# An attention and two mixtures of experts on one core: the first mixture in tiles of 400 rows with the weights stationary

## What is computed

```python
# attention: B=2, H=8, S=768, D=64; queries see only keys of their hash bucket
x = attn_out.transpose(0, 2, 1, 3).reshape(1536, 512)

# first mixture: 8 experts, w1 [8,512,1024], w2 [8,1024,512], the best two for each row
noisy = x @ w_gate + log1p(exp(x @ w_noise)) * noise
top2, top2_w = two best of noisy, their softmax
for e in range(8):
    h = maximum(x[rows of e] @ w1[e], 0)
    out[rows of e] += top2_w * (h @ w2[e])

# second mixture: the same sizes, the best one for each row, fed with the first one's output
```

## Time and profile before

| | |
|---|---|
| median of 3 runs | 950.83 us (947.76 to 951.78) |
| profiled execution | 954.72 us |
| its span, first to last instruction | 953.0 us |
| PE busy | 862.1 us (90%), 4678 matmuls |
| PEld busy | 735.0 us (77%) |
| DVE, ACT, POOL busy | 580.4, 372.7, 399.2 us |
| DMA | 175.12 MB, mean 184 GB/s |

### The profile page before, as it was taken

The page is one execution under the profiler, slowest core; times in us unless marked ns, Lnnn a source line. Parts: engine busy times, 40 slices in busy tenths (PEclk is TensorE's granted clock), DMA queues, the critical chain, the costliest instruction groups (busy, mean ns, idle before and its releaser), DMA issues.

```text
span 953.0 us, 17167 instructions
## 1 busy us (share of the span) xinstructions
PE 862.1 (90%) x4678; PEld 735.0 (77%) x4679; DVE 580.4 (61%) x996; ACT 372.7 (39%) x625; POOL 399.2 (42%) x292
## 2 busy tenths in 40 slices
PE   3899999999984779999999999999886999999991
PEld 2788888888884558888888888887685888888870
DVE  4999999999986834444444444442637544444440
ACT  2778787777883013211112120210431344333003
POOL 2010110101222788642525161644316989896104
PEclk9999999999998779999999999999977899999996
DMA  6678669667884677442525251525586768784118
GB/s 150 134 228 244 163 173 272 207 136 224 250 318 164 212 265 233 166 164 80 173 87 177 67 193 70 175 87 150 149 288 210 274 211 262 224 262 155 44 33 276
DMA packets 101977, 175.12 MB, mean 184 GB/s; under 512 B 35712, under 2 KB 37760, under 8 KB 101952
## 3 DMA queue, kind: packets, MB, share of 16 engines
q1 hardware_dynamic: 66880, 82.79, 29.4%
q10 hardware_dynamic: 28672, 71.05, 23.0%
q0 software_dynamic: 6400, 20.98, 6.6%
HBM read 98.18 MB, written 57.15 MB: 163 GB/s over the span
## 4 chain that ended last, share of the span: by engine, by line
PE 80%; DVE 8%; issue 3%; another core or an unknown queue 3%; DMA 2%; ACT 2%; DVEq 0%; POOLq 0%; POOL 0%; ACTq 0%; SPq 0%
PE bank L1427 8%; PE bank L1429 8%; PE bank L1447 8%; PE bank L1428 8%; PE bank L1449 8%; PE bank L1448 8%; PE bank L1252 7%; PE bank L1458 3%; PE bank L1240 3%; PE bank L1263 3%; PE bank L1264 3%; PE bank L1241 3%; PE bank L1279 2%; PE bank L1409 2%
## 5 line engine op out<-in xcount | busy, mean ns | idle before, releaser
L549 POOL TENSOR_TENSOR wring<-stage,wring 128x1024 f32 (+1 forms) x116 | 274.3, 2401 | 177.7 <-ACT wring L748 171.4
L748 ACT ACTIVATE wring<-stage 128x1024 f32 (+1 forms) x116 | 121.1, 1059 | 372.5 <-PE bank L1429 119.0
L1427 PE MATMUL bank<-wring,xT_hl 128*128 (+1 forms) x352 | 145.3, 413 | 8.3 <-DVE xT_hl L1127 5.8
L1447 PE MATMUL bank<-wring,hT_hl 128*128 (+1 forms) x352 | 142.1, 404 | 4.1 <-DVE hT_hl L1145 4.1
L1429 PE MATMUL bank<-wring,xT_hl 128*128 (+1 forms) x352 | 140.8, 400 | 1.5 <-issue 1.5
L1428 PE MATMUL bank<-wring,xT_hl 128*128 (+1 forms) x352 | 140.8, 400 | 0.0
L1152 DVE COPY work<-bank 128x512 f32<-128x512 f32 x44 | 30.5, 692 | 180.8 <-PE bank L1449 164.5
L1449 PE MATMUL bank<-wring,hT_hl 128*128 (+1 forms) x352 | 138.3, 393 | 0.9 <-issue 0.9
L1448 PE MATMUL bank<-wring,hT_hl 128*128 (+1 forms) x352 | 137.8, 391 | 0.5 <-issue 0.5
L1134 DVE TENSOR_SCALAR work<-bank 128x512 f32<-128x512 f32 x88 | 60.7, 691 | 107.7 <-PE bank L1429 95.7
L890 DVE TENSOR_TENSOR wring<-bank,wring 128x768 fp32r<-128x768 f32 x96 | 91.9, 957 | 11.1 <-ACT wring L666 9.2
(11 more groups left out here) (181 smaller groups left out, 1389.5 us busy)
## 6 DMA issues: line engine op xcount, KB each, us to landing
stage<-in_moe_w_dram ACTq DMA_DIRECT2D x128, 512.0 KB
wring<-wring SPq DMA_DIRECT2D x92, 192.0 KB
ys<-work SPq DMA_DIRECT2D x44, 256.0 KB
work<-xs SPq DMA_DIRECT2D x38, 256.0 KB
xs<-stage SPq DMA_DIRECT2D x8, 1024.0 KB, 5.1
ys<-stage SPq DMA_DIRECT2D x7, 1024.0 KB, 7.2
xs<-stage SPq DMA_DIRECT2D x7, 512.0 KB, 7.9
ys<-stage SPq DMA_DIRECT2D x7, 512.0 KB, 8.0
```

The source lines that it names most:

```text
L549: nc.gpsimd.tensor_tensor(wring[:, bass.ds(at + DC * F, GW)], stage[:, at_stage(g, j), :], wring[:, bass.ds(at, GW)].bitcast(F32), ALU.sub ...
L748: nc.scalar.activation(wring[:, bass.ds(parity * SLOT + high_at(j), GW)], stage[:, j % STAGES, :], ACT.Copy).then_inc(w_high, 1)
L1427: mm(o, xT_hl[:, 0, c, :], wh, start=c == 0, stop=False)
L1447: mm(y_ps[:], hT_hl[:, 0, c, :], wh, start=c == 0, stop=False)
```

## The change

The first mixture gets loops of its own (`wide_experts` on PE and DVE, `wide_load` and `wide_store` on SP). The second keeps its tiles of 128.

- A tile is up to 400 rows of one expert, in blocks of 128, 128, 128 and 16. Rows stand in `xs` and `ys` without gaps; a tile's start row is read from the table `row_of`. What a tile computes beyond its expert's rows is overwritten by the next tile.
- The weights are stationary and the rows move, 400 columns a matmul, in both layers. `up` gives h already turned, so `turn_h` goes. `down` gives y turned, so four transposes for each block (`turn_y`) bring it back, in between the parts of the next `up`.
- In the last tile `down_rows` works block by block with h stationary, 512 columns a matmul, so that the blocks are stored one after the other.
- The ring is three halves (one layer of one expert each); the fourth half's place holds h and x.
- TensorE's code is written out for each of the 8 experts, each with a second copy of the step under a condition, for an expert of more than 400 rows.
- `tables(0)` moves behind the whole first `up`. PE, SP and ACT wait for it there. `gate_weights(0)` moves ahead of it. The first fetches stand at scatters 1, 5, 5 and 5.
- SP loads a whole tile's x with two DMAs, after the four stores of the tile before in its queue; each store waits for the landing of the one before.

In the diff, `wide_load` and `wide_store` are SP's, `high_part` is ACT's, `h_split` and the first `step` DVE's, `up` and the second `step` PE's. `y_out` copies 400 columns of turned y out of PSUM, `x_split` makes high and low of a block, `y_rows` copies 512 columns of y out of PSUM, `down(t, d)` makes 24 matmuls of 400 columns. `XS_TILES` and `YS_TILES` are 28 tiles for the first mixture, before 32 and 31.

```diff
+    WIDE = 400
+    BLOCKS = [min(P, WIDE - at) for at in range(0, WIDE, P)]
+    XS_TILES = [-(-(TOPK[0] * TOK + WIDE) // P), NT[1] + 1]
+        BACK_AT = (1, 3, 5, 6)
-                fetch_at = ((1, 5, 7, 9), (1, 4, 5, 6))[m]
+                fetch_at = ((1, 5, 5, 5), (1, 4, 5, 6))[m]
...
+            def wide_load(t):
+                row = wide_start(t)
+                sp.wait_ge(wide_xmm, t * NB)
+                sp.dma_start(work[:, 3 * DM:6 * DM].rearrange("p (b n) -> p b n", n=DM),
+                             xs_d[0][bass.ds(row, 3 * P)].rearrange("(b p) n -> p b n", p=P)).then_inc(wide_ld, 16)
+                sp.dma_start(wide_rows[3][0:BLOCKS[3]],
+                             xs_d[0][bass.ds(row + 3 * P, BLOCKS[3])]).then_inc(wide_ld, 16)
+            def wide_store(t):
+                row = wide_start(t)
+                for b, n in enumerate(BLOCKS):
+                    sp.wait_ge(wide_yrow, t * NB + (b + 2))
+                    if not (isinstance(t, int) and t == 0 and b == 0):
+                        sp.wait_ge(y_st, t * (16 * NB) + 16 * b)
+                    sp.dma_start(ys_d[0][bass.ds(row + b * P, n)], wide_y[b % 2][0:n]).then_inc(y_st, 16)
+            sp.wait_ge(xs_put, 16 * TT * TOPK[0])
+            sp.wait_ge(rt_tab, 1)
+            wide_load(1)
+            wide_store(0)
+            with sp.Fori(2, NTMIN[0]) as t:
+                wide_load(t)
+                wide_store(t - 1)
...
-            with act.Fori(2, E - 1) as g:
-                high_part(0, g, g, g % 2, table(0, g - 2))
+            for e in range(2, E):
+                high_part(0, e, (downed(e - 2), upped(e - 1)))
...
+                def h_split(t, f):
+                    dve.wait_ge(wide_upped, t * FC + (f + 1))
+                    src = wide_up[f % 3][:, 0:WIDE]
+                    vec.tensor_scalar(wide_h[0][:, f], src, 0.0, None, ALU.max).then_inc(wide_hhigh, 1)
+                    dve.wait_ge(wide_hhigh, t * FC + (f + 1))
+                    vec.scalar_tensor_tensor(out=wide_h[1][:, f], in0=src, scalar=0.0, in1=wide_h[0][:, f].bitcast(F32),
+                                             op0=ALU.max, op1=ALU.subtract).then_inc(wide_hrdy, 1)
+                def step(t, before):
+                    for d in range(DC):
+                        if d == DC - 1:
+                            x_split(t, d)
+                            y_out(before, d)
+                        else:
+                            y_out(before, d)
+                            x_split(t, d)
+                    for f in range(FC):
+                        h_split(t, f)
+                        if f in BACK_AT:
+                            b = BACK_AT.index(f)
+                            y_rows(before, b, wide_back, wide_backed, before * NB + (b + 1))
...
+                def up(t, f, at):
+                    to = wide_up[f % 3][:, 0:WIDE]
+                    for c in range(DC):
+                        high, low = weights(at + (c * F + f * P), P)
+                        mm(to, high, wide_x[0][:, c], start=c == 0, stop=False)
+                        mm(to, high, wide_x[1][:, c], start=False, stop=False)
+                        ins = mm(to, low, wide_x[0][:, c], start=False, stop=c == DC - 1)
+                def step(t, e, before, e_before):
+                    pe.wait_ge(w_low, e_before * GRAN + GRAN)
+                    for d in range(DC):
+                        down(before, d, at)
+                        if d < DC - 1:
+                            turn_x(t, d)
+                        if d == DC - 2:
+                            turn_x(t, d + 1)
+                    pe.wait_ge(w_low, e * GRAN + GRAN // 2)
+                    for f in range(FC):
+                        up(t, f, 2 * e % 3 * HALF_W)
+                        if f in BACK_AT:
+                            turn_y(before, BACK_AT.index(f))
+                for b in range(NB):
+                    turn_x(0, b)
+                for f in range(FC):
+                    up(0, f, 0)
+                pe.wait_ge(rt_tab, 1)
+                for e in range(E):
+                    final = last_tile(e)
+                    if e:
+                        step(before + 1, e, before, e - 1)
+                        with pe.If(final > before + 1):
+                            with pe.Fori(1, WIDE_MAX) as i:
+                                with pe.If(final > before + i):
+                                    step(before + 1 + i, e, before + i, e)
...
+                for b in range(NB):
+                    down_rows(before, b, (2 * E - 1) % 3 * HALF_W)
```

More of the change, by code:

```diff
@@ L46, in lsh_attention_two_moes @@
     STAGES = 4
-    W1H, W1L, W2H, W2L = (i * DC * F for i in range(4))
-    SLOT = 4 * DC * F
+    HALF_W = 2 * DC * F
+    W2H, W2L, W1H, W1L = (i * DC * F for i in range(4))
+    SLOT = 2 * HALF_W
     assert S % (2 * P) == 0 and D == 64 and DC * F == FC * DM and GW == F and H % 2 == 0
@@ L449, in used_tiles, with wide_start @@
                 return sp.value_load(tiles_upto[m][0:1, E - 1:E], min_val=NTMIN[m], max_val=NT[m])
[L451 to L459 removed]
+            def wide_start(t):
+                return sp.value_load(row_of[0:1, bass.ds(t, 1)], min_val=0, max_val=TOPK[0] * TOK)
@@ L460, in _ @@
+            for m in (1,):
+                nt = NT[m]
+                sp.wait_ge(y_back[TT - 1], 16)
+                for t in range(TT):
+                    sp.wait_ge(mixed, t + 1)
+                    keep_x(1, t, 1)
                 slot_x, slot_y = (d[m].rearrange("(t p) n -> t p n", p=P) for d in (xs_d, ys_d))
-                sp.wait_ge(xs_put, 16 * TT * (TOPK[0] + (TOPK[1] if m else 0)))
+                sp.wait_ge(xs_put, 16 * TT * (TOPK[0] + TOPK[1]))
                 def load_x(t):
@@ L615, in _ @@
             pool.wait_ge(w_low, GRAN)
-            low_part(1, 1)
-            with pool.Fori(2, E) as g:
-                low_part(g, g % 2)
+            for e in range(1, E):
+                low_part(0, e)
             pool.wait_ge(rt_tab, 1)
-            low_part(E, 0, range(GRAN // 2))
+            low_part(1, 0, range(GRAN // 2))
             fetch_low()
@@ L724, in _, with high_part @@
             o_copy(2 * H - 1, 1)
-            def high_part(m, e, g, parity, free=None, pieces=range(GRAN)):
+            def high_part(m, e, free=(None, None), pieces=range(GRAN), g=None):
+                g = m * E + e if g is None else g
                 for j in pieces:
@@ L961, in bc, with count_tiles @@
                 return ap.broadcast_to(shape)
+            def count_tiles(m):
+                limits = full_at[:] if m else wide_full
+                n = TT if m else WIDE_MAX
+                link(vec.tensor_tensor(over[:, :, 0:n], bc(cnt[:], [P, E, n], 2), bc(limits, [P, E, n], 1), ALU.is_gt))
+                link(vec.tensor_reduce(ntile[:], over[:, :, 0:n], AX.X, ALU.add))
+                link(vec.tensor_tensor(cumm[:], bc(ntile[:], [P, E, E], 1), tri_in[:], ALU.mult))
+                link(vec.tensor_reduce(cum[:], cumm[:], AX.X, ALU.add))
             def route(m):
@@ L1078, in gate_weights @@
+                vec.scalar_tensor_tensor(out=need[m][:], in0=cum[0:1, E - 2:E - 1].broadcast_to([1, TT]),
+                                         scalar=float((NB, 1)[m]), in1=last_seen[0:1],
+                                         op0=ALU.mult, op1=ALU.add).then_inc(rt_tab, 1)
             def gate_weights(m):
@@ L1197, in _ @@
             route(0)
-            experts(0)
+            wide_experts()
             route(1)
@@ L1405, in turn_x @@
                     else:
-                        pe.wait_ge(x_ld, (t + (1 - FIRST) + loaded) * 16 if m else (t + (1 - FIRST)) * 16)
-                    rows = x_first_in[t] if isinstance(t, int) and t < FIRST else x_in
+                        pe.wait_ge(x_ld, (t + (1 - FIRST)) * 16)
+                    rows = x_first_in[m][t] if isinstance(t, int) and t < FIRST else x_in
                     for c in range(DC):
```

417 lines of the change are left out of this document (298 added, 119 removed).

## The result

The changed kernel takes **971.42 us**, median of 4 runs (968.24 to 983.68), against 949.3 us (946.5 to 951.78) for the kernel before on the same chip: ratio 1.0223, 95% interval 1.0175 to 1.027. It is slower by 2.2%; the interval leaves open whether by more or less than 2%. The forecast was 930 us, with a range of 906 to 952. The profiled execution took 968.24 us, with a span of 966.5.

The account below looks back on a forecast made before the run. TensorE's instruction stream was taken to bound the first mixture. The terms put the last copy of y at 670.2 us, 14.8 earlier; with -6 between the mixtures, -20.8 from the 950.8 median gives 930 us, range 906 to 952.

Parts of the forecast that it names:

- the jumps past the second copies: TensorE's branches over never-run code at eight boundaries: no cost in the sum, considered only in a rival.
- the two unexplained waits: Waits no engine explains, beside POOL's indirect DMAs: 6 us in up(0) (bounds 0, 9), 5 in the last layer (0, 11).
- the first up: Up(0) at the start of the first mixture: 17.3 us, 1.8 for a low-clock start, plus 6 for a wait.
- The wait for x: PE waits for the next tile's x at six boundaries: 3 us each, 18 in all, bounds 0 and 6 each.
- the 3.4: Ahead of the first down, PE restarts at 1.2 GHz after 5.5 us idle and first reads a register: 3.4 us.
- -6 to the logits: Between the mixtures, from the last copy of y to the second gate's logits: 6 us less (-7 to +7).
- The matmuls: First mixture's TensorE stream: 0.180 us per 400-column matmul; matmuls and transposes together 308 us instead of 344.
- The wait for the tables: Between up(0) and the first down, PE stands until rt_tab is ready: 349.4 to 354.9, about 5.5 us.
- 974 us: Rival: TensorE's code comes late at jumps past never-run copies, 8.91 us a boundary, +44 on 930; chance 0.11.
- Free boundaries: Rival: at tile boundaries fast stores and a load hidden under down leave no wait, 912 us; chance 0.25.
- The lost clock: Rival: clock lost at each boundary and between the mixtures, 951 us; chance 0.12 together with milder mixtures of the costs.
- A ninth tile: Rival: an expert over 400 rows adds a tile of 38 us to the first mixture, 968 us; chance 0.02.

Follow-up runs that it names:

- the three edits: Changed kernel without second copies of TensorE's step, next x loaded after the first store, tables(0) computed before the h_split loop: 926.41 us, ratio 0.9758.
- the short jump: Changed kernel with x loaded early, tables early, and each second copy replaced by a condition over 12 never-run matmuls: 930.2 us, ratio 0.9789.
- the early load: Changed kernel with SP issuing the load of the next tile's x behind the first store instead of the fourth: 955.85 us, ratio 1.0000.
- half pace: Changed kernel without second copies, x and tables early, plus a 0.54 us POOL memset after each of fetch_low's 12 gathers: 936.28 us, ratio 0.9864.
- one copy: Changed kernel with the second copies of TensorE's step removed: 962.59 us, ratio 1.0079.
- the early tables: Changed kernel with tables(0) ahead of the h_split loop and gate_weights(0) behind it: 965.63 us, ratio 1.0129.

## Why the prediction was wrong

Two steps of the sum failed. It held the jumps past the second copies at nothing, without a row that said so; they show as 4.3 us ahead of the first `down` and as 8 to 9 us in the six boundaries after it. And it held the two unexplained waits at 6 and 5 us; the first up took 8.7 us longer than the sum with that wait had it, and the last layer 8.1. The wait for x, its largest uncertain term, was not what failed.

The sum put the last copy of y at 670.2 us; it came at 705.58, 35.4 later. By its steps:

| step | predicted | measured | late by |
|---|---|---|---|
| first up starts | 324.3 | 327.14 | 2.8 |
| up(0) | 25.1 | 33.8 | 8.7 |
| from there to the first `down`, with 1.2 of the 3.4 | 6.7 | 13.0 | 6.3 |
| seven tile periods, with 2.2 of the 3.4 for the restart | 287.0 | 296.4 | 9.4 |
| last layer and its copy | 27.1 | 35.2 | 8.1 |

Then -6 to the logits was -4.1 (20.9 us instead of 25.0), and the second mixture took 3.1 less: 34.2 in all on a profiled execution that was forecast at 933.9 and took 968.24. The rest of the 41 us is that this execution lies 3 us below its median, and the one before lay 4 us above its own.

*The matmuls* were right: 0.18 us for 400 columns, and a tile of 224 matmuls in 38.5 us where nothing is late (five times 38.5 with the three edits; 2 x 17.3 + 32 x 0.11 = 38.1 predicted).

*The first up* was priced at 19.1 us and 6 for the first unexplained wait, with 9 as its upper bound; it took 14.7 more than the 19.1. PE has 8.8 us of idling from 340 to 351.6 and 1.1 before it, and it starts again at the low clock a second time, behind the stall:

```profile
327.00:334.00 7.00, 6.86 (x22) 6.89 (x23) 4.53 (x15) 0.00 (x0) 5.48 (x6) 0.55 0.58 217
...
351.60:361.00 9.40, 9.35 (x36) 8.96 (x36) 6.58 (x11) 4.05 (x4) 6.07 (x3) 0.70 0.56 170
```

36 matmuls in 9.4 us where full clock gives 52. I had counted the wait and not the restart behind it. How much of the loss this term is can't be said: with the three edits that stall was 1.84 us, with the short jump there was none, and then x(1) was late instead (gaps of 3.27 and 4.54 us, and of 8.60 and 4.24). x(1) waits for the last scatter, which I did not follow as a bound of its own. So the stall is of another length in every profile, and the 43 us between the spans of the changed kernel and of the three edits have some of it in them.

*The wait for the tables* was foreseen at 5.5 us; it was 6.8 (to 367.8), with one operation of 2.04 us that I took for a small one. The other 6 us are two register reads and the first jump (4.34 us). The prediction's words for this place were "PE starts again at 1.2 GHz after 5.5 us of idling and first reads a register: 3.4": the read is there, and between it and the first matmul stands a jump that the sum does not have.

*The boundaries*: the x part was right in kind and near in size: 11.7 us in six tiles, where 18 stood with the clock in it; the granted clock was 1.00 from 400 to 640 us. That the store order caused it is shown by the early load, which removes it. What the sum held at nothing was the jump. It was among the rivals, at 8.91 us a boundary, from the unexplained wait of the earlier trace rows: that price was wrong, and so was the row (that wait stands beside the train of scatters, and no jump past an unrun copy exists in the kernel before). A jump takes 3.1 to 4.3 us of the sequencer, of which PE shows 0.8 to 2.0 as idle time at each later boundary. That 974 us came out so near is chance: seven jumps at 8.9 stood in for jumps, stalls, tables and x together. The chance of 0.11 was too low for another reason: the prediction itself said that no row shows a way forward past code that was never run; a cost without a row belongs in the sum with its bounds, as the load of x was, and not only among the rivals. The Trainium skill's rule on taken branches (the section named above) had spoken for it.

*The last layer*: 5 us stood for the second unexplained wait, about the middle of its bounds (0 and 11); the piece in the chain is 12.80, and the last layer with its copy was 8.1 us late. In the kernel before, the train stood beside the next-to-last tiles and took about 5 us there.

*The rivals.* Free boundaries (912) are excluded by 11.7 us of waiting on x. The lost clock at the boundaries is excluded: 1.00 granted from 400 to 640 us with 21 us of idling in it. A ninth tile did not come.

What stays open is what slows the issue of instructions beside a long train of indirect DMAs, and why the first up's stall is 1.8 us or none in two of the profiles and 8.9 in the changed kernel's. Pacing the scatters was not tried, so that the scatters cause the stall in the first up is argued from the likeness alone.

## What to carry to other kernels

Count the jumps as you count matmuls: a guard around code that normally does not run is cheap only if that code is short (0.22 us against 3.1 to 5.7 here). Keep the code of the rare case small; putting it behind the common path's end would do as well if the fetch is the cost, but that was not tried. When a new tiling makes TensorE's stream solid, look again at everything that stood beside it for free, first of all the in-order queue that loads the next tile behind the stores of the last. And look at a boundary's rows as well as at the total: with the jumps gone the wait for x grew from 11.7 to 18.2 us there. Do not weigh edits by the spans of single profiles: by these, one copy and the early tables gave 3 us each, the early x 11 and the three together 43, which looks as if each hid the others; by the ratios it was 14, 9 and 21, together 44, and nothing was hidden in the total.

## What was not expected of the hardware

- A taken branch past some 450 instructions that never ran: 3.1 to 5.7 us on TensorE's sequencer; past some 25: 0.22 us. Beside each long one stands a packet of 16 KB on the queue of instructions.
- Beside indirect DMAs issued every 1.26 us, a dozen or more in a row, VectorE stood for 11.3 to 20.1 us at the end of the first mixture in every version without pauses, and TensorE was held up with it, for the most part. At 1.78 us, or with a pause after every third, neither was. A quarter of the bytes did not help.
- TensorE kept its full clock through idle times of 0.4 to 2.8 us, thirteen of them in six tiles, from 400 to 640 us. It had 0.50 right behind an idle time of 8.12 us, but also 0.52 from 685 us in the half pace version behind one of 2.11 us, as in the earlier trace rows behind one of 2.18: the length of the idle time alone does not tell.
